# The second chunk's k turned by VectorE and moved through DRAM, its update five steps later

## The chip, the cores and the metric

The kernel runs on one core of one Trainium2 chip. The metric is the device time of one execution in microseconds (us); the number quoted for a kernel is the median of its runs.

## The reference: what is computed

Three layers, each fed by the one before.

1. A linear attention with decays, for 2 batches and 8 heads of 48 columns over 768 tokens. Per head a 48x48 state is kept. At each token the output is `r_t (state + (u k_t) v_t^T)`, and then the state becomes `w_t state + k_t v_t^T`.
2. A dense feed-forward layer: 1536 tokens, 384 to 2048 columns, ELU, and 2048 back to 384.
3. Four dense experts of 384 to 1024 to 384 with ReLU. Every token goes through all four, and the outputs are summed with the token's normalised probabilities.

Everything is float32 in and out.

## The kernel before, in words

**Tiling.** The 1536 tokens are cut into 12 chunks of 128. Even chunks belong to batch 0, odd ones to batch 1, so chunk 1 is the first of its batch, and its state is first read by chunk 3. The attention of a chunk is done with matrices: decays are multiplied up by scans, k and r are scaled with them (`scale_k`, `scale_r`), scores are formed for all pairs of tokens (`scores`), masked (`mask_scores`) and multiplied with v; `update` multiplies the scaled k, turned so that tokens lie on partitions, with v, and `add_update` adds this to the state. Chunks 0 and 1 are done ahead of everything. The other ten are done beside the first feed-forward layer, whose work is cut into steps `n`. A step is one slice of 128 hidden columns for a tile of tokens: `up(n)`, the ELU on ScalarE and VectorE (`exponential`, `elu`, `hi_g`, `lo_g`), and two steps later `down1(n)`. The first tile is chunks 0 and 1 (256 tokens), steps 0 to 15. Each float32 product is made of three fp32r passes over high and low parts, hence `w_hi`, `w_lo`, `x_hi`, `x_lo`. The low parts of the first layer's weights are made in pieces by GpSimd, and some by VectorE.

**Order.** It is written out by hand, one instruction list per engine with semaphores between them. The dictionaries at the top give the step of each piece: `SCORES` puts chunk 2 at step 8, chunk 3 at 12, chunk 4 at 16, so `old_values`, the values and the update of chunk 2 come at step 10, those of chunk 3 at step 14. `bonus_terms(3)` on GpSimd comes behind nearly all of GpSimd's weight pieces.

**The turned k.** `update(c)` needs the scaled k turned. For chunks 0 and 1 TensorE does it: `turn_k` (L1201) transposes four blocks into a PSUM bank, and ScalarE copies the bank to `kt_sb` (`copy_kt`, L675 on). For chunk 1 both stand in step 0, and `update(1)` in step 2 (L1431), `add_update(1)` in step 3 (L1097). From chunk 2 on VectorE turns k in blocks of 32x32 (`turn_blocks`, L901) into `k_blocks`, and SyncE moves it (`move_blocks`, L453): one DMA writes `k_blocks` to DRAM, SyncE waits until it has landed, and four DMAs read it back in another order into `kt_sb`. `update` waits for all four.

**SyncE's list** issues nearly all DMAs. Ahead of its loop over chunks it holds `load_rkw(3)`, `load_tok(3)`, six weight slices (10 to 15) and `probs`. The loop then is `load_rkw(c)`, `load_tok(c)`, `move_blocks(c - 2)` for c from 4 on. `load_tok(4)` writes over the buffer `tok[1]`, which for chunk 1 also holds the scaled k (`k_of`), and `load_rkw(4)` over `rkw[1]`.

Of the kernel before, what the change touches and what calls it, by code (L numbers as in the profile page):

```python
# [32 lines left out]
P = 128  # L33
# [9 lines left out]
PAIRS = H // 2  # L43
# [22 lines left out]
DEEP = 3  # L66
# [24 lines left out]
SCALE_K = {c: step - 2 for c, step in SCORES.items() if c not in TILE_STARTS} | {FIRST: 5}  # L91
SCALE_R = {c: step - 1 for c, step in SCORES.items() if c > FIRST}
SCALE_R_FIRST = 6

TURNS = {c: step for c, step in SCALE_K.items() if c < NC - B}
LATE_TURNS = {c: SCORES[c] - 1 for c in TILE_STARTS if FIRST < c < NC - B}
# [12 lines left out]
STRIPS = DM // STRIP  # L109
STRIPS_P = P // STRIP  # L110
MOVED = 16 * STRIPS_P
PIECES = 2

HI_FIRST = 6
# [17 lines left out]
def bass_linear_attention_elu_ffn_dense_experts(nc, rkw_d, tok_d, u_d, probs_d, w_d, const_d, out_d):  # L132
    with ExitStack() as ctx:
# [73 lines left out]
        def heads_in(b, first):  # L207
            return b[:, first:first + PAIRS * D]

        def blocks_in(b):  # L210
# [1 line left out]


        BANKS0 = dict(x=bank[6:8], y=bank[2], yt=blocks_in(bank[2]), kt=bank[5], u=heads_in(bank[6], 0), bonus=bank[3])
        BANKS1 = dict(x=bank[0:2], yt=[bank[b][:, 0:P] for b in (4, 3, 5)], kt=bank[7], u=heads_in(bank[7], 0),
                      bonus=bank[5])

        ENDS1 = bank[0:2]
# [208 lines left out]
        @block.sync  # L427
        def _(sp):
            def load_slices(*these):
                for n in these:  # L430
                    sp.dma_start(raw[:, n, :], w_d[n]).then_inc(s_raw[n], 16)

            def load_expert_slice(e, j):
                slot, used = slot_of(e, j), e * PAIRS2 + j // 2 - RING2
                if used < 0:
                    sp.wait_ge(s_down, STEP1 - J1 + slot + 1 + RING)
                else:
                    sp.wait_ge(s_down, STEP1 + used // PAIRS2 * (NT * J2) + (NT - 1) * J2 + used % PAIRS2 * 2 + 2 + RING)
                sp.dma_start(raw[:, slot, :], w_d[J1 + e * J2 + j]).then_inc(s_raw[slot], 16)

            def load_rkw(c):
                need(sp, s_py, c - DEEP + 1)
                need(sp, s_kb, c - DEEP + 1 - FIRST)
                sp.dma_start(rkw[c % DEEP][:, :], rkw_d[c]).then_inc(s_rkw[c % DEEP], 16)

            def load_tok(c):
                need(sp, s_py, c - DEEP + 1)
                need(sp, s_pu, min(c - DEEP + 1, NUPDATE))
                bonus_done(sp, c - DEEP)
                need(sp, s_odd, c - DEEP + 1)  # L450
                sp.dma_start(tok[c % DEEP][:, :], tok_d[c]).then_inc(s_tok[c % DEEP], 16)

            def move_blocks(c):  # L453

                sp.wait_ge(s_kb, c + 1 - FIRST)
                need(sp, s_moved, MOVED * (c - FIRST))
                sp.dma_start(scratch, k_blocks[:, :, :]).then_inc(s_written, 16)
                sp.wait_ge(s_written, 16 * (c + 1 - FIRST))
                sp.wait_ge(s_pu, c)
                for t in range(STRIPS_P):  # L460
                    blocks_t = bass.AP(scratch.tensor, t * P, [[STRIPS_P * P, STRIP], [STRIP * STRIPS_P * P, STRIPS_P], [1, P]])
                    sp.dma_start(kt_sb[t * STRIP:(t + 1) * STRIP, :].rearrange("i (d x) -> i d x", d=STRIPS_P),
                                 blocks_t).then_inc(s_moved, 16)

            def load_decays(c):
                sp.dma_start(rkw[c][:, 2 * NRK:RKW], rkw_d[c][:, 2 * NRK:RKW]).then_inc(s_first[c], 16)

            def load_rk(c):
                sp.dma_start(rkw[c][:, 0:2 * NRK], rkw_d[c][:, 0:2 * NRK]).then_inc(s_rkw[c], 16)

            def load_v(c):
                sp.dma_start(tok[c][:, 2 * DM:3 * DM], tok_d[c][:, 2 * DM:3 * DM]).then_inc(s_tok[c], 16)

            load_decays(0)
            load_rk(0)
            sp.wait_ge(s_zero, 1)
            for o in range(2):
                u_heads = bass.AP(u_d.tensor, o * D, [[1, D], [PD, PAIRS]])
                sp.dma_start(u_col[64 * o:64 * o + D, :], u_heads, allow_slow_non_contiguous=True).then_inc(s_uc, 16)
            load_decays(1)  # L480
            sp.dma_start(const[:, :], const_d).then_inc(s_const, 16)
            load_rk(1)
            load_v(0)
            load_v(1)
            load_slices(0, 1, 2, 3, 4, 5, 6, 7)
            load_rkw(2)
            load_tok(2)
            sp.dma_start(u_rep[:, :], u_d).then_inc(s_u, 16)
            load_slices(8, 9)
            load_rkw(3)  # L490
            load_tok(3)
            load_slices(10, 11, 12, 13, 14, 15)
            sp.dma_start(probs[:, :, :], probs_d).then_inc(s_probs, 16)
            for c in range(4, NC):
                load_rkw(c)
                load_tok(c)
                move_blocks(c - 2)
            for e in range(NE):
                for j in range(J2):
                    load_expert_slice(e, j)  # L500

            with sp.Fori(0, NC - TB) as t:
                store(sp, t)
            for t in range(NC - TB, NC, 2):
                store(sp, t)
            sp.wait_ge(s_out, 16 * NC)
# [168 lines left out]
        def _(act):  # L675
# [117 lines left out]
            for n in range(SINGLE):  # L793
                for c in due(n, 3):
                    hi_x(c, BESIDE["y"])
                exponential(n)
                for c in due(n, 1):
                    copy_odd(c)
                if n == 0:
                    copy_kt(1, BANKS1)  # L800
                for half in HI_BETWEEN.get(n, ()):
                    hi_w_half(*half)
                past = n // J1 - 1
                if n % J1 == LAG - 1 and n > LAG:
                    hi_x2(past, blocks_of(past)[0])
                hi_g(n)
                if n % J1 == LAG - 1 and n > LAG:
                    if past < HALF_TILES:
                        hi_x2_both(past)
                    else:  # L810
                        hi_x2(past, 1)
                        hi_x2(past, 2)
                for c in due(n, 0, ALPHAS):
                    alphas(c)
                    copy_tail(c)
                for c in due(n, 0):
                    scale_state(c)
# [36 lines left out]
        def _(dve):  # L854
# [46 lines left out]
            def turn_blocks(c):  # L901

                dve.wait_ge(s_kp, c + 1)
                need(dve, s_written, 16 * (c - FIRST))
                dve.transpose(k_blocks[:, :, :].rearrange("q t (a j) -> q t a j", a=PAIRS),
                              raw_k(c).rearrange("q (a t i) -> q t a i", a=PAIRS, i=STRIP)).then_inc(s_kb, 1)

            def scale_r(c):

# [151 lines left out]
                dve.tensor_tensor(in_halves(bank[1][:, :]), in_halves(bank[1][:, :]), twice(u3), ALU.add).then_inc(s_c, 1)  # L1061

            for n in range(SINGLE):
                for c in due(n, 1):
                    mask_scores(c, 0, BESIDE)
                    mask_scores(c, 1, BESIDE)
# [28 lines left out]
                        lo_x2(past, 1)  # L1095
                        lo_x2(past, 2)
                if n == 3:  # L1097
                    add_update(1, BANKS1)
                for half in LO_AFTER.get(n, ()):
                    lo_w(*half)  # L1100
                for c in due(n, -1):
# [80 lines left out]
        def _(pe):  # L1182
            def scores(c, banks):
                pe.wait_ge(s_qp, c + 1)
                pe.wait_ge(s_kp, c + 1)
                if banks is BESIDE:
                    pe.wait_ge(s_att, 2 * c)
                    pe.wait_ge(s_x, FIRST)
                    pe.wait_ge(s_sum, 2 * min(c, NUPDATE))
                q, k = q_of(c), k_of(c)  # L1190
                for p in range(PAIRS):
                    cols = slice(p * CH, (p + 1) * CH)
# [15 lines left out]

            def update(c, banks):

                if c < FIRST:
                    pe.wait_ge(s_kt, c + 1)
                else:
                    pe.wait_ge(s_moved, MOVED * (c + 1 - FIRST))
                pe.wait_ge(s_att, c * 2 + 2)
                landed(pe, s_tok, c)
                v = v_of(c)
                for p in range(PAIRS):
                    for i in range(P // STRIP):
                        rows, h = slice(STRIP * i, STRIP * i + STRIP), 2 * p + i // 2  # L1220
                        first = p * P + STRIP * i if c < FIRST else i * P + STRIP * p
                        ins = pe.matmul(banks["u"][rows, p * D:(p + 1) * D],  # L1222
                                        kt_sb[:, first:first + STRIP], v[:, h * D:(h + 1) * D],
                                        start=True, stop=True)
                ins.then_inc(s_pu, 1)
# [17 lines left out]

            def y_free(c):

                pe.wait_ge(s_kt, FIRST)
                pe.wait_ge(s_x, c)

            def turn_bonus(c, yt, first=True):

# [166 lines left out]
            for n in range(SINGLE):  # L1417
# [8 lines left out]
                up(bank[bank_of(n)][:, 0:width(n)], tokens(t), j, n == 0)  # L1426
                if n >= LAG:
                    down1(n - LAG)
                if n == 0:
                    turn_k(1, BANKS1)  # L1430
                if n == 2:  # L1431
                    update(1, BANKS1)
                for c in due(n, 0):
                    scores(c, BESIDE)
# [162 lines left out]
```

## Time and profile before

| | us |
|---|---|
| median of 3 runs (647.87 to 648.05) | 647.96 |
| the profiled execution, its own time | 647.89 |
| its span in the trace | 646.1 |

| engine | busy us | share of the span |
|---|---|---|
| TensorE (PE) | 639.0 | 99% |
| its weight loads (PEld) | 592.0 | 92% |
| VectorE (DVE) | 418.1 | 65% |
| ScalarE (ACT) | 238.2 | 37% |
| GpSimd (POOL) | 295.6 | 46% |

The shares are means over the whole span. The change lies in the first 45 us or so of it, where VectorE is busy for 7 to 9 tenths of each slice, and the DMA engines move some 400 GB/s until about 35 us. The profile's list of a matmul's start and duration models the end: matmuls of 256 columns start every 0.12 us and are given 0.28 us, so starts are compared, not ends.

### The profile page before, as it was taken

The page shows a single profiled execution, that of the slowest core. Times are in us where ns is not written, and L with a number is a line of the kernel's source. Part 1 is how long each engine was busy: PE and PEld are TensorE (multiplying, and loading weights), DVE is VectorE, ACT ScalarE, POOL GpSimd, SP SyncE. Part 2 cuts the span into 40 slices and gives each one's busy share as a digit, 9 for nine tenths or more (in the row PEclk, how much of TensorE's full clock was granted, in tenths as well). Part 3 has the DMA queues.
Part 4 walks back from the last instruction along what each step waited for, and adds up shares of the span by engine and source line. Part 5 has one row for each costly group of instructions (what it writes and reads, how often), then busy time and mean ns, then how long its engine had stood idle before and what let it go on. Part 6 is the DMA issues. An engine that isn't in the chain of part 4 may idle for free.

```text
span 646.1 us, 13797 instructions
## 1 busy us (share of the span) xinstructions
PE 639.0 (99%) x5044; PEld 592.0 (92%) x5044; DVE 418.1 (65%) x786; ACT 238.2 (37%) x561; POOL 295.6 (46%) x370
## 2 busy tenths in 40 slices
PE   8999999999999999999999999999999999999998
PEld 5998999877788888999999999999999999999997
DVE  7888988965357666655565656565656565656564
ACT  4776555645445554222222222222222222222221
POOL 5897424420499999996019900019900019000000
PEclk9999999999999999999999999999999999999999
DMA  8953454300000133100012100012100011001011
GB/s 323 403 196 131 137 167 175 121 18 1 1 2 1 56 102 99 40 1 1 1 50 98 50 1 0 1 49 98 50 1 0 0 50 50 0 1 49 0 50 50
DMA packets 19043, 42.34 MB, mean 66 GB/s; under 512 B 2608, under 2 KB 8752, under 8 KB 18992
## 3 DMA queue, kind: packets, MB, share of 16 engines
q1 hardware_dynamic: 18704, 41.23, 18.5%
q8 instruction: 36, 0.59, 0.4%
q10 hardware_dynamic: 288, 0.39, 0.2%
q14 instruction: 15, 0.12, 0.1%
HBM read 37.16 MB, written 4.46 MB: 64 GB/s over the span
## 4 chain that ended last, share of the span: by engine, by line
PE 89%; POOL 5%; DVE 3%; issue 1%; DMA 0%; ACT 0%; POOLq 0%; DVEq 0%
PE bank L1351 29%; PE bank L1352 28%; PE bank L1353 28%; POOL w_lo L549 4%; PE bank L1197 1%; PE bank L1266 1%; DVE fr L870 1%; PE bank L1278 1%; DMA rkw<-rkw_dram 0%; DVE att L928 0%; DVE fr L889 0%; PE bank L1222 0%; POOL tok L530 0%; DVE bank L1001 0%; PE bank L1286 0%
## 5 line engine op out<-in xcount | busy, mean ns | idle before, releaser
L1351 PE MATMUL bank<-x_lo,w_hi 128*128 128x256 f32 (+2 forms) x416 | 138.2, 332 | 0.6 <-DVE w_lo L971 0.3
L1352 PE MATMUL bank<-x_hi,w_lo 128*128 128x256 f32 (+2 forms) x416 | 135.2, 325 | 0.0
L1353 PE MATMUL bank<-x_hi,w_hi 128*128 128x256 f32 (+2 forms) x416 | 135.2, 325 | 0.0
L1352 PE MATMUL bank<-w_hi,g_lo 128*128 128x384 f32 x384 | 129.6, 337 | 0.0
L1353 PE MATMUL bank<-w_hi,g_hi 128*128 128x384 f32 x384 | 129.3, 337 | 0.0
L1351 PE MATMUL bank<-w_lo,g_hi 128*128 128x384 f32 x384 | 129.0, 336 | 0.0
L833 ACT ACTIVATE g_hi<-bank 128x512 fp32r<-128x512 f32 x96 | 57.5, 599 | 144.3 <-DVE bank L1057 122.4
L1351 PEld LDWEIGHTS bank<-x_lo,w_hi 128*128 128x128 f32 x416 | 78.2, 188 | 10.6 <-issue 2.6
L1353 PEld LDWEIGHTS bank<-x_hi,w_hi 128*128 128x128 f32 x416 | 78.3, 188 | 7.4
L1352 PEld LDWEIGHTS bank<-x_hi,w_lo 128*128 128x128 f32 x416 | 78.3, 188 | 7.1
L1050 DVE TENSOR_TENSOR u_sum<-p_copy,bank 128x256 f32<-128x256 f32 x56 | 23.6, 421 | 92.1 <-ACT p_copy L757 91.4
L561 POOL TENSOR_TENSOR raw<-raw 128x128 f32<-128x128 f32 x16 | 7.4, 460 | 157.8 <-DMA raw<-w_dram 157.8
L1351 PEld LDWEIGHTS bank<-w_lo,g_hi 128*128 128x128 f32 x384 | 72.1, 188 | 0.0
L1353 PEld LDWEIGHTS bank<-w_hi,g_hi 128*128 128x128 f32 x384 | 72.1, 188 | 0.0
L1352 PEld LDWEIGHTS bank<-w_hi,g_lo 128*128 128x128 f32 x384 | 72.0, 187 | 0.0
L757 ACT COPY p_copy<-bank 128x256 f32<-128x256 f32 x56 | 21.0, 374 | 134.4 <-PE bank L1353 134.3
L1135 DVE SCALAR_TENSOR_TENSOR g_lo<-bank,g_hi 128x512 fp32r<-128x512 f32 x96 | 65.8, 685 | 7.1 <-ACT g_hi L833 6.8
L1351 PE MATMUL bank<-g_lo,w_hi 128*128 128x256 f32 (+1 forms) x192 | 65.1, 339 | 0.4 <-DVE x_lo L1017 0.4
L1353 PE MATMUL bank<-g_hi,w_hi 128*128 128x256 f32 (+1 forms) x192 | 64.9, 338 | 0.0
L1352 PE MATMUL bank<-g_hi,w_lo 128*128 128x256 f32 (+1 forms) x192 | 64.7, 337 | 0.0
L1001 DVE SCALAR_TENSOR_TENSOR bank<-neg,bank 128x256 f32<-128x256 f32 (+1 forms) x64 | 35.7, 558 | 36.0 <-ACT neg L771 35.8
L573 POOL TENSOR_TENSOR w_lo<-raw,w_hi 128x768 fp32r<-128x768 f32 x32 | 58.6, 1852 | 0.0
(133 smaller groups left out, 1259.6 us busy)
## 6 DMA issues: line engine op xcount, KB each, us to landing
raw<-w_dram SPq DMA_DIRECT2D x48, 384.0 KB, 3.7
rkw<-rkw_dram SPq DMA_DIRECT2D x10, 772.5 KB, 4.5
tok<-tok_dram SPq DMA_DIRECT2D x10, 576.0 KB, 6.2
k_blocks_dram<-k_blocks SPq DMA_DIRECT2D x8, 256.0 KB, 4.1
kt_sb<-k_blocks_dram SPq DMA_DIRECT2D x32, 64.0 KB, 2.0
out_dram<-acc SPq DMA_DIRECT2D x10, 192.0 KB, 1.9
rkw<-rkw_dram SPq DMA_DIRECT2D x2, 512.0 KB, 4.5
rkw<-rkw_dram SPq DMA_DIRECT2D x2, 260.5 KB, 3.2
```

The lines of the kernel that those rows point to most:

```text
L549: pool.tensor_tensor(w_lo[:, n, part], raw[:, n, part], w_hi[:, n, part].bitcast(F32), ALU.subtract).then_inc(s_wq, 1)
L561: pool.tensor_tensor(s1, a21, a22, ALU.add).then_inc(s_ws, 1)
L573: pool.tensor_tensor(w_lo[:, slot, :], raw[:, slot, :], w_hi[:, slot, :].bitcast(F32), ALU.subtract).then_inc(s_w, 1)
L757: act.copy(p_copy[:, 0, :], bank[6][:, 0:QUARTER]).then_inc(s_pc, 1)
L833: act.activation(g2[0][:, p % 2 * 2 + o, :], bank[o][:, :], ACT.Relu).then_inc(s_gh, 1)
L870: dve.tensor_tensor_scan(fr[:, 0:SCAN], rkw[c % DEEP][:, 2 * NRK:2 * NRK + SCAN], reset[:, :], 0.0, ALU.mult, ALU.add).then_inc(s_f, 1)
L1001: dve.scalar_tensor_tensor(out=h, in0=neg[:, k, 0:w], scalar=-1.0, in1=h, op0=ALU.add, op1=ALU.max).then_inc(s_elu, 1)
L1050: dve.tensor_tensor(u2, p1, p6, ALU.add).then_inc(s_u2, 1)
L1135: dve.scalar_tensor_tensor(out=g2[1][:, r, :], in0=bank[o][:, :], scalar=0.0, in1=g2[0][:, r, :].bitcast(F32), op0=ALU.max, op1=ALU.subtra ...
L1351: pe.matmul(out, wh, ml, start=start, stop=False, skip_group_check=shared)
L1352: pe.matmul(out, wl, mh, start=False, stop=False, skip_group_check=shared)
L1353: return pe.matmul(out, wh, mh, start=False, stop=stop, skip_group_check=shared)
```

## The change

Chunk 1's k goes the way of chunks 2 to 9. `turn_k(1)` and `copy_kt(1)` are gone; `turn_blocks(1)` stands on VectorE in step 3, where `add_update(1)` was. `move_blocks(1)` stands on SyncE behind `probs` and ahead of the loop. `update(1)` is on TensorE behind the matmuls of step 7, and `add_update(1)` on VectorE at the head of step 8. The counts of `s_kb`, `s_written` and `s_moved` are shifted by one chunk, `load_rkw(4)` now waits for `turn_blocks(1)`, the sum of chunk 1 lies in bank 5 instead of bank 7, and so the values of chunk 2 wait for `add_update(1)`, while the scores of chunk 2 no longer do.

```diff
+UPDATE_1 = 7
+TURNED = 1
-        BANKS1 = dict(x=bank[0:2], yt=[bank[b][:, 0:P] for b in (4, 3, 5)], kt=bank[7], u=heads_in(bank[7], 0),
+        BANKS1 = dict(x=bank[0:2], yt=[bank[b][:, 0:P] for b in (4, 3, 5)], u=heads_in(bank[5], 0),
 def load_rkw(c):
-                need(sp, s_kb, c - DEEP + 1 - FIRST)
+                need(sp, s_kb, c - DEEP + 1 - TURNED)
 def move_blocks(c):
-                sp.wait_ge(s_kb, c + 1 - FIRST)
-                need(sp, s_moved, MOVED * (c - FIRST))
+                sp.wait_ge(s_kb, c + 1 - TURNED)
+                need(sp, s_moved, MOVED * (c - TURNED))
                 sp.dma_start(scratch, k_blocks[:, :, :]).then_inc(s_written, 16)
-                sp.wait_ge(s_written, 16 * (c + 1 - FIRST))
+                sp.wait_ge(s_written, 16 * (c + 1 - TURNED))
             sp.dma_start(probs[:, :, :], probs_d).then_inc(s_probs, 16)
+            move_blocks(1)
             for c in range(4, NC):
                 load_rkw(c)
                 load_tok(c)
                 move_blocks(c - 2)
...
-                if n == 0:
-                    copy_kt(1, BANKS1)
 def turn_blocks(c):
-                need(dve, s_written, 16 * (c - FIRST))
+                need(dve, s_written, 16 * (c - TURNED))
-                              raw_k(c).rearrange("q (a t i) -> q t a i", a=PAIRS, i=STRIP)).then_inc(s_kb, 1)
+                              k_of(c).rearrange("q (a t i) -> q t a i", a=PAIRS, i=STRIP)).then_inc(s_kb, 1)
 VectorE, step n
+                if n == UPDATE_1 + 1:
+                    add_update(1, BANKS1)
...
                 if n == 3:
-                    add_update(1, BANKS1)
+                    turn_blocks(1)
 TensorE
 def scores(c, banks):
-                    pe.wait_ge(s_sum, 2 * min(c, NUPDATE))
+                    pe.wait_ge(s_sum, 2 * (c - 1) if c == FIRST else 2 * min(c, NUPDATE))
 def update(c, banks):
-                if c < FIRST:
+                if c < TURNED:
                     pe.wait_ge(s_kt, c + 1)
                 else:
-                    pe.wait_ge(s_moved, MOVED * (c + 1 - FIRST))
+                    pe.wait_ge(s_moved, MOVED * (c + 1 - TURNED))
+                if c == 1:
+                    pe.wait_ge(s_x, FIRST)
 def y_free(c):
-                pe.wait_ge(s_kt, FIRST)
                 pe.wait_ge(s_x, c)
+                if c == FIRST:
+                    pe.wait_ge(s_sum, 2 * c)
 step n
-                if n == 0:
-                    turn_k(1, BANKS1)
-                if n == 2:
+                if n == UPDATE_1:
                     update(1, BANKS1)
```

## Rows read from the trace of the kernel before

**Rows 1.** The page: the PEclk line of the slices, and the chain by line.

```profile
PEclk9999999999999999999999999999999999999999
...
PE bank L1351 29%; PE bank L1352 28%; PE bank L1353 28%; POOL w_lo L549 4%; PE bank L1197 1%; PE bank L1266 1%; DVE fr L870 1%; PE bank L1278 1%; DMA rkw<-rkw_dram 0%; DVE att L928 0%; DVE fr L889 0%; PE bank L1222 0%; POOL tok L530 0%; DVE bank L1001 0%; PE bank L1286 0%
```

**Rows 2.** The chain of waits, 46 to 70 us: start, us, what.

```profile
49.04 0.92 POOL tok L530
...
66.83 0.32 DVE x_lo L1017
```

**Rows 3.** Timeline of TensorE, 18 to 24 us: start, us, engine, line, out<-in, count.

```profile
18.51 0.28 PE L1353 MATMUL bank<-x_hi,w_hi 128*128 128x256 f32 x1
18.63 0.60 PE L1206 MATMUL bank<-const,tok 128*128 128x128 f32 x4
...
19.19 0.28 PE L1352 MATMUL bank<-x_hi,w_lo 128*128 128x256 f32 x1
...
22.33 0.28 PE L1353 MATMUL bank<-g_hi,w_hi 128*128 128x256 f32 x1
22.54 0.55 PE L1222 MATMUL bank<-tok,kt_sb 128*32 128x48 f32 x32
...
23.24 0.29 PE L1352 MATMUL bank<-x_hi,w_lo 128*128 128x256 f32 x1
23.36 0.28 PE L1353 MATMUL bank<-x_hi,w_hi 128*128 128x256 f32 x1
```

**Rows 4.** Timeline of VectorE, 27 to 38 us.

```profile
27.13 0.73 DVE L937 TENSOR_TENSOR st<-bank,st 64x192 f32<-64x192 f32 x2
...
32.81 0.71 DVE L905 STREAM_TRANSPOSE k_blocks<-rkw 128x512 f32<-128x512 f32 x1
...
37.87 0.43 DVE L1001 SCALAR_TENSOR_TENSOR bank<-neg,bank 128x256 f32<-128x256 f32 x1 [0.89 <-ACT neg L771]
```

**Rows 5.** Timeline of SyncE's DMA issues, 20 to 40 us.

```profile
20.62 0.43 SPq L493 DMA_DIRECT2D probs<-probs_dram  x1
...
23.18 0.33 SPq L451 DMA_DIRECT2D tok<-tok_dram  x1
33.55 0.33 SPq L457 DMA_DIRECT2D k_blocks_dram<-k_blocks  x1
37.98 1.75 SPq L462 DMA_DIRECT2D kt_sb<-k_blocks_dram  x4
```

**Rows 6.** Issues by line: count, KB each, us from issue to landing; last, all writes of L457.

```profile
probs<-probs_dram SPq DMA_DIRECT2D x1, 24.0 KB, 12.7
...
tok<-tok_dram SPq DMA_DIRECT2D x1, 576.0 KB, 14.1
...
k_blocks_dram<-k_blocks SPq DMA_DIRECT2D x1, 256.0 KB, 4.4
kt_sb<-k_blocks_dram SPq DMA_DIRECT2D x4, 64.0 KB, 2.0
...
DMA to landing us min/median/max: 2.0/4.1/5.7
```

**Rows 7.** Timeline of TensorE, 33 to 68 us; in brackets idle time and what ended it.

```profile
33.76 0.29 PE L1351 MATMUL bank<-x_lo,w_hi 128*128 128x256 f32 x1
...
43.06 0.52 PE L1222 MATMUL bank<-tok,kt_sb 128*32 128x48 f32 x32
...
48.69 1.10 PE L1197 MATMUL bank<-rkw 48*64 48x128 f32 x32 [0.65 <-DVE rkw L912]
...
52.39 0.36 PE L1351 MATMUL bank<-x_lo,w_hi 128*128 128x256 f32 x1 [0.28 <-DVE w_lo L971]
...
58.81 0.28 PE L1353 MATMUL bank<-g_hi,w_hi 128*128 128x256 f32 x1
59.18 0.39 PE L1351 MATMUL bank<-x_lo,w_hi 128*128 128x256 f32 x1
...
61.30 0.28 PE L1353 MATMUL bank<-g_hi,w_hi 128*128 128x256 f32 x1
61.62 1.10 PE L1197 MATMUL bank<-rkw 48*64 48x128 f32 x32
...
67.19 0.38 PE L1351 MATMUL bank<-g_lo,w_hi 128*128 128x256 f32 x1 [0.36 <-DVE x_lo L1017]
```

More of the change, by code:

```diff
@@ L1220, in update @@
                         rows, h = slice(STRIP * i, STRIP * i + STRIP), 2 * p + i // 2
-                        first = p * P + STRIP * i if c < FIRST else i * P + STRIP * p
+                        first = p * P + STRIP * i if c < TURNED else i * P + STRIP * p
                         ins = pe.matmul(banks["u"][rows, p * D:(p + 1) * D],
```

## The prediction

> **What bounds the kernel now.** I read the page first. TensorE is busy for nearly the whole span, and the chain of waits gives 85% of the span to the three lines of matmul passes [rows 1]. So from some point on the end moves with TensorE one for one. The chain in order of time says from where: before 67 us it doesn't run through TensorE, but through GpSimd's weight pieces and `bonus_terms` until about 50 us and then through VectorE, whose last link is `x_lo` at 66.83 us [rows 2]. From 67.19 us on it is TensorE alone. TensorE's timeline says how close the two are. In the first 67 us it stands still only briefly, each time for VectorE: before 48.69, 52.39, 59.18, 61.62 and 67.19 us [rows 7]. What TensorE gains before 48 us is lost in these waits; what it loses there is taken up by them until they are used up. Their sum is the main number of this case.
>
> By starts, with 0.12 us as the distance between starts of such matmuls (23.24 and 23.36 [rows 3]): a bracketed idle time counts from a modelled end that lies 0.28 us behind the start, so 0.16 us is to be added. Before 52.39 us this gives 0.28 + 0.16 = 0.44, before 67.19 us 0.36 + 0.16 = 0.52. The scores at 48.69 us give 0.65 + 0.16 = 0.81; a change to small matmuls costs 0.21 between starts instead of 0.12 (22.33 to 22.54 [rows 3]), so 0.72. The other two: 59.18 - 58.81 - 0.12 = 0.25, and 61.62 - 61.30 - 0.21 = 0.11 [rows 7]. Slack in all: 0.72 + 0.44 + 0.25 + 0.11 + 0.52 = 2.04 us.
>
> **Removed: `turn_k(1)` and ScalarE's copy.** From 18.51 to 19.19 us there are 0.68 us where two distances would be 0.24, so the four transposes cost TensorE 0.44 us [rows 3]. The copy is on ScalarE, off the chain. Both gains lie ahead of a wait that VectorE sets, so taken alone they move the end by 0 (at most 0.44, if VectorE were not the bound).
>
> **`update(1)` from step 2 to step 7.** It costs the same in both places: 22.33 to 23.24 is 0.91, less two distances 0.67 us, there and here between two groups of big matmuls [rows 3]. TensorE, 0.44 + 0.67 ahead of before less what VectorE takes back in steps 3 to 6 (its low parts are then barely ready), would come to it a little before 33.76 us, where `up(8)` starts now [rows 7]; I take 33.5.
>
> **`turn_blocks(1)` for `add_update(1)` on VectorE, step 3.** 0.71 us for 0.73 us, start 27.13 us [rows 4]: nothing. Without that equality an excess of it would go into the chain, as VectorE has no gap there. `add_update(1)` at the head of step 8 meets a gap: VectorE waits 0.89 us for ScalarE before 37.87 us [rows 4], and the 0.73 fit if `update(1)` is done by about 37.0. If it is not, VectorE stands, and behind it stand `elu(8)`, the scan of chunk 3 and the masks of chunk 2.
>
> **The move, which decides.** No row shows this write at this place, so I work it out and bound it. `turn_blocks(2)` starts at 32.81 and SyncE issues its write at 33.55 us, 0.74 later [rows 4, 5]; chunk 1's write is so issued at 27.13 + 0.74 = 27.9 us. Ahead of it in SyncE's queue are the weight slices and `probs`, issued at 20.62 and landed 12.7 us later, at 33.3 [rows 5, 6]. Now look at chunk 2's write: issued at 33.55, landed at 33.55 + 4.4 = 37.95, while the `tok` load issued ahead of it at 23.18 landed at 23.18 + 14.1 = 37.3 [rows 5, 6]. It landed 0.65 us behind the load ahead of it, 14 us old, so the queue is served in order and the write waits its turn. Chunk 1's write is then down at 33.3 + 0.65 = 33.95 us. The four reads are issued over 1.75 us, one each 0.43 us, so the last starts 1.3 us in and lands 2.0 us later [rows 5, 6]: 33.95 + 1.3 + 2.0 = 37.25 us. Bounds: with a write at its fastest, 2.0 us from issue [rows 6], the blocks are there at 27.9 + 2.0 + 3.3 = 33.2 us; with its slowest 5.7 us on top of the 33.3, at 42.3. I take 37.2, since the row of chunk 2 is the same situation six us later. Without the `rkw` and `tok` loads of chunk 4 behind them the last slices may land up to 1 us sooner; hence 36.2 as the near end of my own case.
>
> TensorE waits at `update(1)` from 33.5 to 37.2, 3.7 us, and everything behind it in its list waits. `up(8)` starts 0.5 us later (22.54 to 23.24 is 0.70, less one big matmul and its slow first distance, about 0.2 [rows 3]), at 37.7 instead of 33.76: TensorE is 3.9 us late.
>
> **How much of that is taken up.** VectorE becomes late too, but less: what it waits for is fed by TensorE, at most 3.9 late, and it had a gap of 0.89 there [rows 4], so `elu(8)` is late by 3.0 at most, and by less behind it, where it isn't fed by TensorE step by step. GpSimd, whose weight pieces don't depend on this, isn't late at all. So TensorE is the later one at each of the five waits, and each goes in full. 3.9 - 2.04 = 1.9 us are left at 67 us, and from there TensorE has no idle time to give. The sum for the profiled execution: 647.89 + 1.9 = 649.8. The median is 0.07 above that execution, which changes nothing in it.
>
> **What else is moved past.** In SyncE's list `load_rkw(4)` goes from 21 to about 36 us and `load_tok(4)` behind `update(1)`, to 38: both are first used in step 12, behind 45 us, hidden. `move_blocks(2)` goes behind `load_tok(4)`: write at about 38.5, landed within 4.4 to 5.7 us [rows 6], blocks there 3.3 us later, at 46.2 to 47.5; `update(2)` on TensorE is due at 43.06 + 3.9 = 47.0 [rows 7]. So 0, at worst 0.5 us more. The new waits of chunk 2's values and `load_rkw(4)` are long fulfilled.
>
> **Two rules against the trace.** The Trainium skill, "DMA: Bandwidth & Descriptors", section "Anatomy of one DMA", gives a DMA some 2 us fixed and bytes over 436 GB/s. For 256 KB this estimate is 2.6 us from issue, blocks there at 33.8 us, stall 0.3, and no loss. The trace has 4.4 us for such a write behind a full queue. The same page, section "Queues, rings and completion order", says that an engine consumes its ring in order, which is what the two landings show; by it the write waits for the slices.
>
> The granted clock is full in every slice [rows 1]; the longest stand of TensorE in the rows is 0.65 us [rows 7]. The skill's "TensorE: Matmul & The Clock Gate", "Part 1: The HAM clock gate", says that an idle array falls to 1.2 GHz. That would be a second loss, below.
>
> **Rivals.**
> 1. *The clock falls in the stall.* New here is an idle time of 3.7 us; no row shows one. If TensorE then ran at half its clock for as long as it had stood, half of 3.7 us, 1.85, is lost on top, all of it after the slack: 651.7. Against it: the stall is short, and weights and matmuls are dense on both sides. Chance 0.12.
> 2. *The transfer comes in time, or nearly: not slower.* If the write doesn't queue behind the slices, or these land by 31.5 us without the loads behind them, the blocks are there by 35.3 or sooner, TensorE is late by at most 2.0 us, and the five waits take all of it. It decides at a write landed by 32.0 us. For it: the stretch to 67 us hangs on GpSimd and VectorE, not TensorE. Against it: the landing of `probs` at 33.3. Time 647.9, and the removed transposes do not show either. Chance 0.17, and 0.10 more for a half-way case at 648.6.
> 3. *VectorE takes its delay on into its chain*, so that less than 2.04 is absorbed, as `add_update(1)` and `elu(8)` hold up scans and masks. Its waits before 48 us speak for it; that TensorE would still be the later one at 48.69, 52.39 and 59.18 speaks against. All of the 3.9 stay at the worst: 651.8; a half of the slack lost gives 650.8. Chance 0.05.
> 4. *Faster*, by transposes gone and a smoother start: up to 0.44 us, which is no difference that can be told. By over 0.2%, chance 0.02.
>
> **How the numbers follow.** My forecast, 649.8, has a chance of 0.54, with its own range of 648.8 to 650.4. About 0.2%, 1.3 us, is what a measurement of this kernel can tell from no change. The likeliest case lies mostly beyond it, rivals 1 and 3 wholly: slower 0.68. Rival 2 and a margin of the forecast are within it: same 0.30; faster 0.02. The range from 647.8 to 651.5 leaves out the worst of rivals 1 and 3.
>
> **What would show it.** In the changed profile: a wait of TensorE at L1222 (`update`) for the DMA into `kt_sb`, some 3.7 us, near 33.5 us; the write issued near 27.9 and the reads near 34.0; the five waits of [rows 7] gone; `update(2)` without a wait; the granted clock still 1.00 between 37 and 45 us. The forecast is wrong if the reads start before 32, if TensorE still waits for VectorE at 48 to 67 us, or if the clock is down.

## The result, and the profile after

| | before | after |
|---|---|---|
| median of 6 runs, us | 647.83 (647.74 to 648.05) | 653.98 (652.32 to 654.30) |
| ratio, 95% interval | | 1.0088 (1.0078 to 1.0099) |
| the profiled execution, us | 647.89 | 653.93 |
| its span, us | 646.1 | 652.1 |
| mean granted clock | 1.000 | 0.994 |

Slower by 6.2 us, where 649.8 was forecast and 651.5 was the end of the range. The direction and the place were right; the size was not. On the page of the changed kernel two lines stand out against [rows 1]: a slice whose granted clock is 7 tenths, and two DMA pieces in the chain.

```profile
PEclk9979999999999999999999999999999999999999
...
PE bank L1357 28%; PE bank L1358 28%; PE bank L1359 28%; DMA k_blocks_dram<-k_blocks 2%; PE bank L1200 1%; DVE fr L871 1%; DMA kt_sb<-k_blocks_dram 1%; DVE bank L1002 1%; PE bank L1272 1%; DVE att L929 1%; DVE fr L890 1%; PE bank L1284 1%; ACT neg L772 0%; PE bank L1227 0%; ACT g_hi L780 0%
```

**The stall.** TensorE's timeline, changed kernel: the last matmul of step 7, `update(1)`, the first three of `up(8)`, the scores of chunk 2, the first of `up(9)`. The rows answer to the first of [rows 7].

```profile
32.87 0.28 PE L1359 MATMUL bank<-g_hi,w_hi 128*128 128x256 f32 x1
37.84 0.87 PE L1227 MATMUL bank<-tok,kt_sb 128*32 128x48 f32 x32 [4.69 <-DMA kt_sb<-k_blocks_dram]
38.63 0.58 PE L1357 MATMUL bank<-x_lo,w_hi 128*128 128x256 f32 x1
39.02 0.42 PE L1358 MATMUL bank<-x_hi,w_lo 128*128 128x256 f32 x1
39.23 0.41 PE L1359 MATMUL bank<-x_hi,w_hi 128*128 128x256 f32 x1
...
42.77 1.47 PE L1200 MATMUL bank<-rkw 48*64 48x128 f32 x32
44.17 0.38 PE L1357 MATMUL bank<-x_lo,w_hi 128*128 128x256 f32 x1
```

The reader is to see 4.69 + 0.16 = 4.85 us of standing at `update(1)`, and `up(8)` at 38.63 instead of 33.76: 4.87 us late. SyncE's issues of the changed kernel say where the blocks were, against [rows 5]:

```profile
27.77 0.33 SPq L459 DMA_DIRECT2D k_blocks_dram<-k_blocks  x1
34.40 1.74 SPq L464 DMA_DIRECT2D kt_sb<-k_blocks_dram  x4
...
39.26 0.38 SPq L459 DMA_DIRECT2D k_blocks_dram<-k_blocks  x1
43.95 1.75 SPq L464 DMA_DIRECT2D kt_sb<-k_blocks_dram  x4
```

The write took 34.40 - 27.77 = 6.6 us. In the chain of waits of the changed kernel it is the longest piece, and it is followed by the reads and by TensorE:

```profile
27.77 6.61 DMA k_blocks_dram<-k_blocks
...
35.71 2.08 DMA kt_sb<-k_blocks_dram
37.84 0.87 PE bank L1227 x32
```

**The clock.** Windows of TensorE in the changed kernel: stretch, its length, busy us (instructions), granted clock, DMA share, GB/s.

```profile
34.00:36.00 2.00, 0.00 (x0) 1.00 0.13 39
36.50:37.00 0.50, 0.00 (x0) 0.75 0.34 100
37.00:37.50 0.50, 0.00 (x0) 0.50 1.67 258
38.00:40.00 2.00, 2.00 (x38) 0.50 1.05 374
43.50:44.00 0.50, 0.50 (x24) 0.92 0.01 4
```

TensorE had been standing since 33 us when the granted clock fell between 36.5 and 37.0 to 0.5, the lower of its levels, 1.2 GHz; it was back at 2.4 near 43.6. In between matmuls start every 0.21 us (39.02, 39.23) instead of 0.12. From `up(8)` to `up(9)` it took 44.17 - 38.63 = 5.54 us, and from the start of `update(1)` to `up(8)` 38.63 - 37.84 = 0.79 us. In the kernel before, the first `up` behind `update(1)` (which starts at 22.54 [rows 3]) and `up(9)` start here:

```profile
23.02 0.39 PE L1351 MATMUL bank<-x_lo,w_hi 128*128 128x256 f32 x1
...
37.05 0.39 PE L1351 MATMUL bank<-x_lo,w_hi 128*128 128x256 f32 x1
```

so the same pieces took 37.05 - 33.76 = 3.29 and 23.02 - 22.54 = 0.48 us. The low clock cost 2.25 us behind `up(8)` and 0.31 at the update, 2.56 in all, and TensorE was 44.17 - 37.05 = 7.12 us late. The spans differ by 6.0: only 1.1 us was taken up behind it.

The low clock did not cost the same in every run. Of the six runs of the changed kernel, four have a mean clock of 0.994 or 0.995 and took 653.9 to 654.3 us; two have 0.997 and took 652.3 and 652.8. No trace of those two was kept. The kept traces with 0.997, of four kernels below, show the lower level for 3.4 us, where the one above shows it for 6.8; so those two runs most likely had the shorter stretch.

**VectorE.** Its timeline in the changed kernel has a wait that the prediction did not have. The second transpose may not write `k_blocks` before the first chunk's write has left it:

```profile
27.04 0.70 DVE L906 STREAM_TRANSPOSE k_blocks<-tok 128x512 f32<-128x512 f32 x1
...
34.48 0.71 DVE L906 STREAM_TRANSPOSE k_blocks<-rkw 128x512 f32<-128x512 f32 x1 [2.49 <-DMA k_blocks_dram<-k_blocks]
...
41.83 0.43 DVE L1002 SCALAR_TENSOR_TENSOR bank<-neg,bank 128x256 f32<-128x256 f32 x1 [2.31 <-ACT neg L774]
```

`elu(8)` moved from 37.87 [rows 4] to 41.83, 4.0 us.

Four questions follow: is late placement harmless in itself; is the clock's share 2.56; does VectorE's wait count; and why was so little of the delay taken up.

### The profile page after: what moved, and what is told of

Its sections match the earlier page's. It is cut to its first block, busy times and chain, and to the rows that moved or that the text cites. A ratio compares the mean times of both kernels' runs of the same rounds, so it can differ in the third digit from the quotient of the medians.

```text
span 652.1 us, 13798 instructions
## 1 busy us (share of the span) xinstructions
PE 640.8 (98%) x5040; PEld 593.9 (91%) x5040; DVE 419.2 (64%) x787; ACT 238.0 (37%) x560; POOL 293.4 (45%) x370
## 4 chain that ended last, share of the span: by engine, by line
PE 87%; DVE 5%; DMA 3%; ACT 2%; issue 1%; SPq 0%; POOL 0%; DVEq 0%; ACTq 0%; POOLq 0%
PE bank L1357 28%; PE bank L1358 28%; PE bank L1359 28%; DMA k_blocks_dram<-k_blocks 2%; PE bank L1200 1%; DVE fr L871 1%; DMA kt_sb<-k_blocks_dram 1%; DVE bank L1002 1%; PE bank L1272 1%; DVE att L929 1%; DVE fr L890 1%; PE bank L1284 1%; ACT neg L772 0%; PE bank L1227 0%; ACT g_hi L780 0%
```

## The experiments

Eleven kernels, in four groups that each shared a chip with the kernel before.

| kernel | median us | range | before, same chip | ratio, 95% |
|---|---|---|---|---|
| late update and sum alone | 647.28 | 647.15 to 647.37 | 647.77 | 0.9992 (0.9983 to 1.0002) |
| changed, matmuls in the stall | 651.33 | 650.91 to 652.28 | 647.77 | 1.0053 (1.0036 to 1.0070) |
| changed, four slices behind the move | 653.44 | 651.82 to 654.34 | 647.77 | 1.0092 (1.0075 to 1.0109) |
| changed, own buffer for chunk 1 | 653.15 | 652.10 to 654.64 | 647.77 | 1.0091 (1.0074 to 1.0108) |
| changed, matmuls and own buffer | 651.37 | 650.98 to 651.78 | 647.86 | 1.0051 (1.0035 to 1.0068) |
| changed, two moves ahead (seven of its eight runs) | 650.80 | 648.43 to 651.36, see below | 647.86 | 1.0033 (1.0020 to 1.0046) |
| before, 17 extra matmuls | 648.87 | 648.74 to 649.76 | 647.86 | 1.0017 (1.0007 to 1.0026) |
| before, 34 extra matmuls | 650.51 | 650.49 to 650.55 | 647.86 | 1.0040 (1.0026 to 1.0055) |
| changed, write issued by ScalarE | 652.36 | 651.92 to 652.95 | 647.74 | 1.0074 (1.0057 to 1.0091) |
| before, sum alone late | 647.26 | 647.23 to 647.54 | 647.74 | 0.9993 (0.9984 to 1.0003) |
| changed, three moves ahead | 647.80 | 647.58 to 649.32 | 647.82 | 1.0006 (0.9997 to 1.0016) |

### Late placement alone

```diff
+                if n == 7:
                     update(1, BANKS1)
+                if n == 8:
+                    add_update(1, BANKS1)
```

TensorE and ScalarE still turn k in step 0; bank 5 and the waits are those of the change.

> One part of the change alone, on the kernel before: the update of chunk 1 stands behind step 7 and its state sum at the head of step 8, in bank 5 and with the changed waits, but TensorE still turns the k and ScalarE still copies it, in step 0. Theory (the stall for the DMA blocks and the low clock behind it are the whole loss): nothing waits, so 647.8, within 0.5. Rival (putting update and sum late, with the loads of chunk 4 and the move of chunk 2 behind them in SyncE's list, costs by itself): 649 or more, with a wait at the update of chunk 2.

647.28: nothing of the loss is here, though TensorE waits 0.42 us for the blocks at the update of chunk 2. It is even 0.5 us below the kernel before, which neither theory had; the runs of the two do not overlap (at most 647.37, at least 647.71), but the interval of the ratio holds 1. More on that below.

### Matmuls in the stall

```diff
                 if n == UPDATE_1:
+                    for _ in range(36):
+                        pe.matmul(bank[7][:, 0:256], w_hi[:, 0, 0:P], x_hi[:, 0, 0:256], start=True, stop=True)
                     update(1, BANKS1)
```

> The changed kernel, with 36 extra matmuls of 256 columns (36 x 0.12 = 4.3 us) into the unused bank 7 just ahead of the update of chunk 1, inside the stall of 4.85 us. They compute nothing that is used. Theory: the stall stays, the granted clock stays at full, and the 2.25 us that steps 8 took longer at half clock are gone: 654.0 - 2.25 = 651.7 (within 0.5). Rival (the clock's loss is hidden by waits behind it, the late VectorE sets the end): 653.5 or more, at full clock.

651.33, with a granted clock of 1.00 in all four runs, against 653.98 for the changed kernel. The profiled run still waits, for what the extra matmuls leave over (waits of TensorE, 17 to 80 us: total, times, longest):

```profile
PE bank L1227 <- DMA kt_sb<-k_blocks_dram: 1.2, 1, 1.2
```

So keeping TensorE busy, with work that is thrown away, gives back 2.6 us by the medians: 2.8 against the four runs at 0.994 and 0.995 (median 654.2), 1.2 against the two at 0.997 (652.6). That is the clock, about as the timeline had it (2.56, in a run at 0.994). In the profiled run the blocks even came 1.0 us later (`update(1)` at 38.81, not 37.84), and the span is still 1.7 us shorter. What is left, 651.33 - 647.77 = 3.6 us, is the stall.

### Four slices behind the move

```diff
-            load_slices(10, 11, 12, 13, 14, 15)
-            sp.dma_start(probs[:, :, :], probs_d).then_inc(s_probs, 16)
+            load_slices(10, 11)
             move_blocks(1)
+            load_slices(12, 13, 14, 15)
+            sp.dma_start(probs[:, :, :], probs_d).then_inc(s_probs, 16)
```

> The changed kernel, with the move of chunk 1 ahead of weight slices 12 to 15 and probs in SyncE's list, so that its write has only the slices up to 11 before it. These landed at 29.1 us, so the write lands at about 29.8 and the blocks at 33.1; TensorE is there at 33.0. Theory (queue order): stall below 0.5 us, full clock, 647.9. Rival (the write takes 6.6 us from issue whatever is ahead of it): blocks at 37.8 as before, 654. Rival (VectorE's wait at the second transpose sets the loss): that wait shrinks too, but the late slices would now hold ScalarE: above 649.

Right about the write, wrong about the time. SyncE's issues of this kernel:

```profile
27.71 0.33 SPq L459 DMA_DIRECT2D k_blocks_dram<-k_blocks  x1
30.14 1.74 SPq L464 DMA_DIRECT2D kt_sb<-k_blocks_dram  x4
...
35.32 0.66 SPq L459 DMA_DIRECT2D k_blocks_dram<-k_blocks  x1
44.16 1.75 SPq L464 DMA_DIRECT2D kt_sb<-k_blocks_dram  x4
```

Chunk 1's write landed in 2.4 us instead of 6.6. But the four slices and the loads of chunk 4 now came in one pile ahead of chunk 2's write, which took 8.8 us. TensorE's waits, 17 to 80 us:

```profile
PE bank L1228 <- DMA kt_sb<-k_blocks_dram: 4.4, 2, 4.0
```

4.0 of the 4.4 us are at the update of chunk 2, and the granted clock fell there too (0.89 over 48 to 64 us), though only at 48.2 us, when TensorE had been at work again for 0.7 us. The stall had moved, with its clock.

### An own buffer for chunk 1

```diff
+        def turned_in(c):
+            if c == 1:
+                return bonus_v_sb[:, :, :].rearrange("p a d -> p (a d)")[:, 0:PAIRS * P].rearrange("p (t x) -> p t x", t=STRIPS_P)
+            return k_blocks[:, :, :]
-                need(dve, s_written, 16 * (c - TURNED))
-                dve.transpose(k_blocks[:, :, :].rearrange(...
+                need(dve, s_written, 0 if c == 2 else 16 * (c - TURNED))
+                dve.transpose(turned_in(c).rearrange(...
```

> The changed kernel, with chunk 1 turned into a part of bonus_v_sb that is free by then, instead of k_blocks, so that VectorE's transpose of chunk 2 no longer waits for the write of chunk 1 (2.49 us of idle time in the changed kernel). Theory (TensorE's stall and clock set the loss, VectorE's wait lies beside the stall): unchanged, 653.5 to 654.2. Rival (VectorE's wait is what is carried down its chain to 77 us): 2 us or more less, at most 652.

> The changed kernel with both earlier edits at once: 36 extra matmuls inside the stall, and chunk 1 turned into a part of bonus_v_sb, so that VectorE's second transpose does not wait. Theory (what is left with a full clock is TensorE's stall alone): as with the matmuls alone, 650.9 to 652.3. Rival (VectorE's wait of 2.5 us, covered by the clock's loss before, now shows): 1 us or more below the kernel with the matmuls alone.

VectorE's wait of 2.5 us for the write was gone in both. Alone, 653.15 with runs from 652.1 to 654.6, over those of the changed kernel (652.3 to 654.3): no difference that these runs can tell, if just below the range of the theory. With the extra matmuls, which keep the clock at 1.00 in seven of the eight runs of the two kernels (the eighth shows 0.949 and took 651.35, no longer than the others), 651.37 against 651.33: none. The wait lay beside the stall; what replaced it is a wait of 2.1 to 2.3 us for the update's result at the head of step 8. The rivals fall.

### How much of a delay is taken up

```diff
                 if n == 2:
                     update(1, BANKS1)
+                if n == 7:
+                    for _ in range(17):    # or 34
+                        pe.matmul(bank[7][:, 0:256], w_hi[:, 0, 0:P], x_hi[:, 0, 0:256], start=True, stop=True)
```

> The kernel before with 17 extra matmuls of 256 columns into the unused bank 7 behind step 7: TensorE 17 x 0.12 = 2.0 us late there, at full clock, nothing else changed. They compute nothing that is used. The prediction's slack (five waits, 2.04 us in all, take the delay up): 647.8 to 648.1. Rival (ScalarE and VectorE are fed by TensorE's up step by step, so they get late too and the waits do not close): 648.8 to 649.8, half or more of the delay at the end.

> As the one with 17, but with 34 extra matmuls, 4.0 us. The prediction's slack: 647.8 + 4.0 - 2.04 = 649.8. Rival (the waits do not close): 650.8 to 651.5.

2.0 us late in step 7 gave 648.87 - 647.86 = 1.0 at the end, and 4.0 gave 650.51 - 647.86 = 2.65. So 1.0 and 1.35 us were taken up at the end, not 2.04, in kernels with no wait for the blocks and a full clock. The first time is the rival's; the second lies between theory (649.8) and rival (650.8 and more). TensorE's timeline with 17 extra matmuls shows what became of the waits (the scores of chunk 3, and the two places that answer to 59.18 and 67.19 in [rows 7]):

```profile
49.94 1.10 PE L1197 MATMUL bank<-rkw 48*64 48x128 f32 x32
...
60.10 0.39 PE L1351 MATMUL bank<-x_lo,w_hi 128*128 128x256 f32 x1 [0.27 <-DVE x_lo L954]
...
68.10 0.39 PE L1351 MATMUL bank<-g_lo,w_hi 128*128 128x256 f32 x1 [0.36 <-DVE x_lo L1017]
```

The first wait gave its 0.72 (49.94 is 1.25 later than 48.69, of 2.0). By 60.10 TensorE is 0.92 late, by 68.10 0.91, and the last wait is exactly as long as before, 0.36. TensorE has come down to VectorE's own delay, and can come down no further. The wait at 67.19 did not close in the changed kernel either:

```profile
72.97 0.39 PE L1357 MATMUL bank<-g_lo,w_hi 128*128 128x256 f32 x1 [0.37 <-DVE x_lo L1018]
```

VectorE's delay has two parts. The first comes from TensorE. ScalarE can begin a step's `exponential` only when TensorE has done that step's `up`; a late `up(11)` makes the rest of ScalarE's list late, and VectorE's next two `elu` stand behind it. The chain of waits with 17 extra matmuls goes this way:

```profile
46.85 0.39 ACT neg L769
...
50.57 0.44 DVE bank L1001
```

The second part comes later, from instructions that take longer. VectorE's rows, first before, then with 17 extra matmuls, then in the changed kernel:

```profile
50.45 0.42 DVE L1001 SCALAR_TENSOR_TENSOR bank<-neg,bank 128x256 f32<-128x256 f32 x1
51.65 0.59 DVE L971 TENSOR_TENSOR w_lo<-raw,w_hi 128x384 fp32r<-128x384 f32 x1
...
57.14 0.71 DVE L889 TENSOR_TENSOR_SCAN fr<-rkw,inv_end 128x260 f32<-128x260 f32 x1
```

```profile
50.57 0.43 DVE L1001 SCALAR_TENSOR_TENSOR bank<-neg,bank 128x256 f32<-128x256 f32 x1
...
51.78 0.94 DVE L971 TENSOR_TENSOR w_lo<-raw,w_hi 128x384 fp32r<-128x384 f32 x1
...
57.63 1.14 DVE L889 TENSOR_TENSOR_SCAN fr<-rkw,inv_end 128x260 f32<-128x260 f32 x1
```

```profile
55.73 0.43 DVE L1002 SCALAR_TENSOR_TENSOR bank<-neg,bank 128x256 f32<-128x256 f32 x1 [0.41 <-ACT neg L774]
...
62.48 1.15 DVE L890 TENSOR_TENSOR_SCAN fr<-rkw,inv_end 128x260 f32<-128x260 f32 x1
```

At `elu(12)`, the first row of each, VectorE is 0.12 us late with 17 extra matmuls, 2.11 with 34 (52.56), and 5.28 in the changed kernel, where TensorE had been 1.96, 3.95 and 7.12 late between `up(8)` and `up(9)`. So each time 1.84 us, or nearly the 2.04 of the prediction, had been taken up by then. After that the same instructions took longer in all three kernels: the scan 1.14 or 1.15 instead of 0.71, and with 17 extra matmuls `w_lo` 0.94 instead of 0.59. That added 0.8, 0.5 and 0.5 us to VectorE's delay by about 60 us of the kernel before. The rival's number, 648.8 to 649.8, was met with 17 extra matmuls, but of the 1.0 us its mechanism brought only 0.12; that hit is luck. With 34 it brought most.

### Two moves, then three moves ahead

```diff
-            load_slices(10, 11, 12, 13, 14, 15)
+            load_slices(10, 11)
             move_blocks(1)
+            load_slices(12, 13)
+            move_blocks(2)
+            load_slices(14, 15)
+            load_rkw(4)
+            load_tok(4)
+            sp.dma_start(probs[:, :, :], probs_d).then_inc(s_probs, 16)
             for c in range(5, NC):
+                if c == 5:                 # the second of the two kernels only
+                    move_blocks(3)
                 load_rkw(c)
                 load_tok(c)
```

> The changed kernel with SyncE's list in another order: slices 10 and 11, the move of chunk 1, slices 12 and 13, the move of chunk 2, slices 14 and 15, the loads of chunk 4, probs. Both writes now have little ahead of them: chunk 1's blocks at about 33.7, chunk 2's write issued at 33.6, its blocks at about 40, before 43.1. Theory (the whole loss is a write behind a full queue, the stall, and the clock behind it): no stall over 0.7 us, full clock, 647.3 to 648.0. Rival (moving through DRAM so early costs in itself, by VectorE's transpose or by late slices): above 649.

650.80, so wrong as worded. The stalls at chunks 1 and 2 were down to 0.78 us and none, but the loads of chunks 4 and 5 had piled up ahead of chunk 3's write, which took 10.5 us to land:

```profile
59.50 0.55 PE L1232 MATMUL bank<-tok,kt_sb 128*32 128x48 f32 x32 [3.34 <-DMA kt_sb<-k_blocks_dram]
```

Its runs fall in two kinds: five at a clock of 0.997 took 650.6 to 651.4 us, two at 0.999 and 1.000 took 648.4 and 648.5; no trace of those two was kept, so whether they stood at chunk 3 is not known. (An eighth took 1261.8 us, for a reason no trace shows; median and ratio leave it out.)

> The kernel with the two moves ahead (slices 10, 11, move of chunk 1, 12, 13, move of chunk 2, 14, 15, loads of chunk 4, probs), and now also the move of chunk 3 ahead of the loads of chunk 5. There the stall had gone on to the update of chunk 3 (3.34 us), behind the loads of chunks 4 and 5 that had piled up. Theory (a write behind a full queue is the whole loss, wherever it lands): chunk 3's blocks at about 52, before the 56 at which they are wanted, no stall over 0.8 us, full clock, 647.3 to 648.3. Rival (the extra trip through DRAM cannot be fitted in; the pile-up moves on to chunk 4, or the late loads of chunk 5 hold VectorE): 649 or more.

647.80 against 647.82. SyncE's issues around the third move, and all of TensorE's waits from 17 to 130 us:

```profile
45.48 0.33 SPq L459 DMA_DIRECT2D k_blocks_dram<-k_blocks  x1
49.42 1.75 SPq L464 DMA_DIRECT2D kt_sb<-k_blocks_dram  x4
```

```profile
PE bank L1365 <- DVE w_lo L980: 0.6, 1, 0.6
PE bank L1365 <- DVE x_lo L1026: 0.4, 1, 0.4
PE bank L1365 <- DVE g_lo L1016: 0.4, 1, 0.4
PE bank L1365 <- DVE x_lo L973: 0.2, 1, 0.2
```

None is for the blocks. Every part of the change is in this kernel, only the order of SyncE's loads differs, and its time is that of the kernel before. Its ten runs are not of one kind: five lie at 647.6, below every run of the kernel before on that chip (647.75 and more), and three at 649.0 to 649.3, at full clock; what varies there stays open.

### The write on another queue

```diff
 ScalarE, step 4
+                if n == 4:
+                    act.wait_ge(s_kb, 1)
+                    act.dma_start(scratch, k_blocks[:, :, :]).then_inc(s_written, 16)
```

> The changed kernel, with the write of chunk 1's blocks to DRAM issued by ScalarE in step 4 (at about 27.8 us) instead of by SyncE; the four reads stay with SyncE. Theory (on SyncE's queue the write waits for the weight slices issued before it, on a queue of its own it does not): the write lands by 31, not 34.4; the reads, still behind the slices, land at 34 to 35.5; the stall falls from 4.85 to between 1 and 2.5 us, the clock stays full or nearly, 648 to 649.5. Rival (the DMA engines are full with slices whatever the queue): write at 34 again, 653 to 654.

Mostly the rival, though its 653 to 654 was not reached. DMA issues of this run, 26 to 40 us (count, KB, us to landing):

```profile
k_blocks_dram<-k_blocks ACTq DMA_DIRECT2D x1, 256.0 KB, 5.7
```

5.7 us instead of 6.6, a stall of 3.7, the clock down all the same, 652.36. A queue of its own was worth 0.9 us to the write; fewer slices on the way (2.4 us to landing, above) were worth 4.2. In both kernels the share of the 16 DMA engines is at or near 1.0 until 32.0 us, and 0.14 and 0.08 from 33.0 to 33.5. So the write waits above all for traffic that was issued ahead of it, on whichever queue, and much less because of its place in its own queue; that it is the full engines that hold it up fits these rows, and no run takes them apart from the memory behind them.

### The sum alone

```diff
-                if n == 3:
-                    add_update(1, BANKS1)
+                if n == 8:                 # at its head
+                    add_update(1, BANKS1)
```

> The kernel before with only VectorE's state sum of chunk 1 moved from step 3 to the head of step 8 (its sum in bank 5); TensorE's update stays in step 2. The late update alone gave 647.28 against 647.8. Theory (that gain is VectorE's: 0.7 us taken out of its unbroken stretch of steps 3 to 7 and put into its gap before step 8): 647.1 to 647.5. Rival (the gain is TensorE's, whose update moved to step 7): 647.8.

647.26, as with the update moved too: the gain of the first experiment, as far as there is one (this interval also holds 1, and the runs again do not overlap), is VectorE's, not TensorE's. The sum's other bank and the moved waits are in both kernels, and no run takes them apart. In this kernel VectorE comes to chunk 2's `scale_r` and bonus earlier, and the sum fills the gap ahead of `elu(8)`, now at 36.50 instead of 37.87:

```profile
27.01 0.69 DVE L889 TENSOR_TENSOR_SCAN fr<-rkw,inv_end 128x260 f32<-128x260 f32 x1
...
35.26 0.55 DVE L944 TENSOR_REDUCE bonus_sb<-tok 128x8 f32<-128x384 f32 x1
35.73 0.73 DVE L937 TENSOR_TENSOR st<-bank,st 64x192 f32<-64x192 f32 x2
36.50 0.43 DVE L1001 SCALAR_TENSOR_TENSOR bank<-neg,bank 128x256 f32<-128x256 f32 x1
```

Of 1.4 us gained there 0.7 reached the span (645.4). Not all of the 1.4 is the moved sum: the scan behind its old place took 0.69 us here and 1.13 before. Further on VectorE waits 1.0 us for GpSimd's `bonus_terms(3)`. These two kernels, 647.28 and 647.26, are the fastest of the study and below both kernels of the case.

## Why the prediction was wrong, point by point

**What bounds the kernel: right.** The first 67 us hang on GpSimd and VectorE, the rest on TensorE alone. The sum moved into VectorE's gap seems to have gained 0.5 us; the transposes taken from TensorE (in the kernel with three moves ahead) show no gain.

**`turn_k` and the copy gone, `update(1)` and `add_update(1)` moved: right at 0**, with one thing missed. Taking `add_update(1)` out of step 3 gained some 0.5 us where nothing was put in its place (647.28, 647.26), and none by the median with the transpose there (647.80; the faster half of those runs is at 647.6). That the transpose used the gain up is argued, since the moves differ too. The row with the gap of 0.89 us stood in [rows 4], and I used it only as a cover.

**The move: right in mechanism, too small.** A stall of 3.7 was forecast, 4.85 came. Without the clock's 0.31 at the update, `up(8)` was 4.56 us late, where 3.9 was forecast. TensorE was ready at 32.99, not 33.5; the write landed at 34.40, not 33.95; the reads took 3.4 us, not 3.3. "The queue is served in order" was only the smaller half of the reason: on a queue of its own the write still took 5.7 us of 6.6. The figure of the Trainium skill, "DMA: Bandwidth & Descriptors", section "Anatomy of one DMA", is given for DMAs that GpSimd issues, and this one is SyncE's. My estimate by it, 2.6 us for this write, is near the write with four slices fewer ahead (2.4 us) and far from the one in the changed kernel (6.6).

**VectorE's wait for `k_blocks`: missed.** "The new waits of chunk 2's values and `load_rkw(4)` are long fulfilled" left out that of `turn_blocks(2)`, 2.49 us. It cost nothing measurable.

**"TensorE is the later one at each of the five waits, and each goes in full": refuted.** This is one of the two steps that failed. I added five waits of TensorE to a slack of 2.04 us and took VectorE for the engine in time; the rows at 59.18 and 61.62 do not even name it as what ended the wait. The waits are the distance to VectorE, and VectorE was late itself: TensorE still waited 0.37 us for it at the place of the last wait. A pure delay of 2.0 us had 1.0 taken up, one of 4.0 had 1.35, the change's 7.12 had 1.1. The size of the slack was nearly right, 1.84 by VectorE's `elu(12)`; what was missing is that VectorE's scan then takes 1.15 us instead of 0.71. That left TensorE 5.78 us late at the last wait (72.97 against 67.19), and 0.2 more came behind it. Rival 3, with a chance of 0.05, had VectorE carrying its delay on, but through `add_update(1)`, `elu(8)` and the scans and masks held up by them, not through a longer scan.

**The clock: the other step.** Rival 1 had the mechanism and a price of 1.85, and a chance of 0.12. It cost 2.56 by the timeline and 2.6 by experiment, where the forecast had nothing. The rule of the Trainium skill, "TensorE: Matmul & The Clock Gate", section "Part 1: The HAM clock gate", that an idle array falls to 1.2 GHz, is what this trace shows between 36.5 and 37.0 us. The argument against it, that weights and matmuls are dense on both sides, did not count.

**The sum with the measured terms:** 4.56 late at `up(8)`, + 2.56 for the clock, - 1.1 taken up, = 6.0, the difference of the spans. Against the forecast's 3.9, + 0, - 2.04 these are 0.7, 2.6 and 0.9 us more. The range failed as three errors of one sign came together and I had treated them as rivals that exclude each other.

## What to carry to other kernels

A wait for DMA in front of a busy TensorE is charged twice if it lasts: once as itself and once in the clock behind it. Work out where the transfer stands among the traffic, not only what it takes alone, and if loads are put behind it, see whose transfer they then pile up in front of.

Waits of the bounding engine are slack only as far as the engine it waits for stays in time, and it does not if it is fed by the first, or if its own instructions take longer once they are shifted against the others. To know the slack, delay the engine by a known amount and look at the end.

A gap in an otherwise unbroken list of the engine that feeds the chain can be worth an instruction that is moved into it: here 0.73 us of work moved brought `elu(8)` 1.4 us forward and the median 0.5, which the interval can just not tell from nothing.

## What the runs showed of the hardware

- The granted clock fell to 0.5 in five profiled runs with one long stall each. With idle times of 4.7 and 4.4 us (as the rows give them) it fell while TensorE stood; with 4.0, 3.7 and 3.3 us it fell 0.7, 0.1 and 0.6 us after TensorE had begun to work again. It stayed full over the 1.2 us that extra matmuls had left.
- The low level lasted 6.8 us in the first of these and 3.4 us in the other four. The changed kernel's runs with a mean clock of 0.994 or 0.995 took 653.9 to 654.3 us, those with 0.997 652.3 and 652.8.
- At the lower level matmuls of 256 columns started every 0.21 us instead of every 0.12.
- A write of 256 KB to DRAM landed 2.4 us from issue with little ahead of it, 5.7 us on a queue of its own beside a loaded one, 6.6 us behind the slices, 8.8 us behind slices and the loads of one chunk, and 10.5 us behind slices and the loads of two.
- The same scan of 260 columns on VectorE takes 1.13 us in the kernel before, 0.69 us without the sum ahead of it and 0.66 us in the changed kernel, with the transpose ahead of it; and a later one 1.14 or 1.15 us instead of 0.71 in the delayed kernels. Each time GpSimd's work beside it moves the other way: its eight `w_lo` pieces took 6.87 us beside the scan of 1.13 and 7.45 beside the one of 0.69; its two instructions L526 1.15 us beside the scan of 1.14 and 1.87 beside the one of 0.71. No run here tells why.

```profile
27.89 1.13 DVE L889 TENSOR_TENSOR_SCAN fr<-rkw,inv_end 128x260 f32<-128x260 f32 x1
```
